# Eight zero blocks issued from ACT's queue instead of SP's, in a fused attention, routed-expert and gated-projection kernel

## The reference

```python
# 1. gated recurrence over 768 steps for 4 x 8 heads of width 40
C = f_stab * C + i_stab * outer(v_t, k_t);  n = f_stab * n + i_stab * k_t
y_t = sigmoid(o_t) * (C @ q_t) / max(|n . q_t|, 1)
# 2. x = y as 3072 tokens x 320; one of 8 experts a token
logits = x @ w_gate;  e_idx = argmax(logits)
out[mask_e] = gate_w * sigmoid(x @ w_output_gate)[e] * (relu(x[mask_e] @ w1[e]) @ w2[e])   # 320 -> 1024 -> 320
# 3. RMS norm, then (silu(xn @ w_gate) * (xn @ w_val)) @ w_out                              # 320 -> 1536 -> 320
```

## Time and profile before

| | us |
|---|---|
| median of 3 runs (863.89 to 868.11) | 866.64 |
| the profiled execution's own time | 862.2 |
| its span, first to last instruction | 860.4 |
| PE busy | 824.9 (96%) |
| DVE busy | 516.9 (60%) |
| ACT busy | 389.3 (45%) |
| POOL busy | 152.1 (18%) |

### The profile page before, as it was taken

One profiled execution on the slowest core, in us unless ns is written; L12 is line 12 of the kernel. 1 busy time (PEld: TensorE's weight loads), 2 busy tenths in 40 slices (PEclk: granted clock), 3 DMA queues, 4 the chain that ended last, 5 costly groups with the idle time before them and its releaser, 6 DMA issues.

```text
span 860.4 us, 18327 instructions
## 1 busy us (share of the span) xinstructions
PE 824.9 (96%) x6220; PEld 742.1 (86%) x6221; DVE 516.9 (60%) x1086; ACT 389.3 (45%) x727; POOL 152.1 (18%) x234
## 2 busy tenths in 40 slices
PE   6999998897999999999999999999999999999994
PEld 3878777696999999999998898888888888888883
DVE  5489876897787787887873353354353354354331
ACT  5455553553777777777752322323223233233221
POOL 3557775630000000000100001001001001001001
PEclk8799998798999999999999999999999999999998
DMA  6667778598989988899921001000100100100000
GB/s 186 147 179 210 209 216 217 179 316 259 298 256 278 284 260 281 250 278 285 321 87 45 1 1 50 19 0 31 37 0 30 37 0 30 37 0 30 1 1 30
DMA packets 74605, 115.72 MB, mean 134 GB/s; under 512 B 10920, under 2 KB 43208, under 8 KB 74552
## 3 DMA queue, kind: packets, MB, share of 16 engines
q1 hardware_dynamic: 71864, 106.37, 42.0%
q0 software_dynamic: 2688, 8.68, 2.8%
HBM read 97.18 MB, written 17.83 MB: 134 GB/s over the span
## 4 chain that ended last, share of the span: by engine, by line
PE 87%; DVE 4%; DMA 3%; issue 2%; SPq 2%; POOL 1%; ACT 0%; POOLq 0%; ACTq 0%; DVEq 0%
PE psum L1556 46%; PE psum L1678 5%; PE psum L1677 5%; PE psum L1676 5%; PE psum L1628 4%; PE psum L1630 4%; PE psum L1629 4%; PE psum L1499 3%; PE psum L1454 3%; PE psum L1475 2%; PE psum L1522 2%; PE psum L1469 1%; PE psum L1513 1%; PE psum L1655 1%; PE psum L1548 1%
## 5 line engine op out<-in xcount | busy, mean ns | idle before, releaser
L1412 DVE TENSOR_TENSOR gated_lo<-gated,gated_hi 128x512 fp32r<-128x512 f32 x72 | 49.9, 693 | 182.2 <-ACT gated_hi L929 182.2
L924 ACT ACTIVATE sigm_sb<-psum 128x512 f32<-128x512 f32 x72 | 43.1, 598 | 249.6 <-PE psum L1556 249.6
L1556 PE MATMUL psum<-nT_hi,w_gv_hi 128*128 128x512 f32 x432 | 122.2, 391 | 1.8 <-DVE nT_lo L1399 1.8
L1556 PE MATMUL psum<-nT_lo,w_gv_hi 128*128 128x512 f32 x432 | 122.0, 391 | 0.0
L1556 PEld LDWEIGHTS psum<-nT_lo,w_gv_hi 128*128 128x128 f32 x432 | 81.2, 188 | 17.8
L754 POOL DMA_INDIRECT out<-out_rows,slot_idx x24 | 23.2, 968 | 389.4 <-ACT out_rows L935 384.0
L1556 PEld LDWEIGHTS psum<-nT_hi,w_gv_hi 128*128 128x128 f32 x432 | 78.6, 188 | 14.4 <-issue 2.1
L1676 PE MATMUL psum<-w_out_hi,gated_hi 128*128 128x320 f32 x288 | 89.2, 310 | 0.0
L1678 PE MATMUL psum<-w_out_hi,gated_lo 128*128 128x320 f32 x288 | 89.1, 309 | 0.0
L1677 PE MATMUL psum<-w_out_lo,gated_hi 128*128 128x320 f32 x288 | 89.0, 309 | 0.0
L1556 PE MATMUL psum<-nT_hi,w_gv_lo 128*128 128x512 f32 x288 | 88.7, 389 | 0.0
(11 more groups left out here) (225 smaller groups left out, 1588.3 us busy)
## 6 DMA issues: line engine op xcount, KB each, us to landing
w_raw<-w SPq DMA_DIRECT2D x38, 640.0 KB, 6.4
w_raw<-w SPq DMA_DIRECT2D x38, 512.0 KB, 4.4
w_raw<-w SPq DMA_DIRECT2D x76, 128.0 KB, 5.0
kv_tok<-tok SPq DMA_DIRECT2D x24, 324.0 KB, 6.1
qk_sb<-qk SPq DMA_DIRECT2D x48, 160.0 KB
x_tile<-x_by_expert SPq DMA_DIRECT2D x12, 386.0 KB, 3.1
y_sorted<-y_tile SPq DMA_DIRECT2D x12, 323.0 KB, 5.2
og_tok<-o_tok SPq DMA_DIRECT2D x24, 160.0 KB, 5.7
```

What stands on the lines that cost most here:

```text
L924: nc.scalar.activation(sigm_sb[f % 2][:], bank[2 * (f % 2)][:], ACT.Sigmoid).then_inc(sig_ready, 1)
L1412: dve.tensor_tensor(gated_lo[f % 4][:], gated[f % 2][:], gated_hi[f % 4][:].bitcast(F32), ALU.subtract).then_inc(hv_lo, 1)
L1556: m = mm(dst, w, x, start=(n == 0), stop=(n == len(terms) - 1))
```

## The change

The eight zero blocks, with the load of the count that each of them needs, leave SP's program and stand in ACT's, between `gate_exp(NC - 1)` and `e_step(0)`. ACT waits for `zero_made` and `cnt_table` ahead of them. What they write, the tile they read and the semaphore `zero_rows` that they increment are the same, and SP's waits for `tables_ready`, `zero_rows` and the scatters stay.

```diff
             x_load(1, TE, row)
             w2_load(1, ex)
-            sp.wait_ge(cnt_table, 1)
-            for e in range(E):
-                n_e = sp.value_load(cnti[0:1, e:e + 1], min_val=0, max_val=NTOK)
-                sp.dma_start(x_by_expert[bass.ds(n_e + e * RS, TE), :].rearrange("(s p) n -> p s n", p=P),
-                             zero[:].unsqueeze(1).to_broadcast([P, TE // P, XW])).then_inc(zero_rows, 16)
             sp.wait_ge(tables_ready, 2)
             sp.wait_ge(zero_rows, 16 * (E + TE // TS))
             rows_scattered(NC - 1)
...
             h_high(0, 0, TE)
             gate_exp(NC - 1)
+            act.wait_ge(zero_made, 2)
+            act.wait_ge(cnt_table, 1)
+            for e in range(E):
+                n_e = act.value_load(cnti[0:1, e:e + 1], min_val=0, max_val=NTOK)
+                act.dma_start(x_by_expert[bass.ds(n_e + e * RS, TE), :].rearrange("(s p) n -> p s n", p=P),
+                             zero[:].unsqueeze(1).to_broadcast([P, TE // P, XW])).then_inc(zero_rows, 16)
```

## The result

The changed kernel takes 872.79 us (median of 10 runs, 868.43 to 877.78) where the kernel before, run beside it, takes 863.75 (860.80 to 868.66). The ratio is 1.0085 with a 95% interval of 1.0062 to 1.0108, so the change costs 7.3 us (5.4 to 9.3). The two medians lie 9.0 us apart, also inside that interval; every cost in this document is worked out from its ratio. The profiled execution took 868.43 us.

A forecast was written before the change was run, and what follows sets the result against it. PE, without idle time from 214 to 430 us, was taken to bound the kernel; 9.7 us of later SP less 1.6 of clock gave 8.1, added to 866.64: forecast 874.7 us, range 870.5 to 881.5.

The forecast's parts named there:

- The loop on ACT as long as SP's, 11.83 us: ACT's eight loads and issues ahead of h_high(0,1) take what SP's took, 11.83 us.
- DVE late by 12.3 us: DVE finishes h_low(0,3) at 197.3 instead of 185.05, so the tables behind it are ready at 206.7.
- SP late by 12.3 - 2.63 = 9.7: SP's wait before tile 2's loads ends 9.7 us later; the threshold, 2.63 us, is how early the tables had been.
- PE's pauses, and the 9.7 us of the sum: New pause of about 10 us in expert_out(0); last pause, before tile 2's work, shrinks to 1.5, ending 9.7 later.
- The clock holds behind the last pause, 1.6 us back: Behind a last pause of only 1.5 us, PE keeps its full clock, which gives back 1.6 us.
- Nothing gives it back: PE's unbroken stretch behind its last pause has no idle time to absorb the delay: 8.1 us later in all.
- the prediction's other branch: PE's clock falls all the same behind the last pause: 876.3 us.
- The rival of a dearer issue on ACT: ACT's issues cost up to POOL's 1008 ns, lengthening the loop by up to 5.1 us: 876.3 to 881.4; chance 0.20.
- The rival of an ACT that isn't held: Issuing is short on ACT or its arithmetic goes on beside it, so the time stays 866.6; chance 0.06.
- with all loads at 272 ns the loop is 1.7 us shorter: Lower bound on ACT's loop: 8 x (479 - 272) = 1.7 us below SP's 11.83.
- The 9.3 us of transfer: Eight zero blocks of 386 KB at 331 GB/s: 9.3 us of transfer, beside 11.83 us of issuing.
- rival 3: In between: a loop of 5 to 8 us on ACT, lateness 2 to 6 us, 869 to 873; chance 0.09.

The follow-up runs named there:

- act_busy: The kernel before, blocks left on SP, with 24 chained copies on ACT where the changed kernel has the blocks; ratio 1.0069 (1.0043 to 1.0095).
- act_busy4: The kernel before, blocks left on SP, with 4 chained copies on ACT where the changed kernel has the blocks; ratio 0.9990 (0.9968 to 1.0012).
- act_busy12: The kernel before, blocks left on SP, with 12 chained copies on ACT where the changed kernel has the blocks; ratio 1.0004 (0.9980 to 1.0028).
- w1_first: First half of tile 2's first weights loaded ahead of the zero-row wait: on the kernel before, ratio 0.9938; on the changed kernel, 1.0081.
- hoist_act: The changed kernel with the eight register loads in a row first, then the eight issues, all on ACT; ratio 1.0095 (1.0058 to 1.0131).
- half_each: The changed kernel with four of the blocks on ACT at the same place and four on SP; ratio 1.0022 (0.9995 to 1.0050).
- act_late: The changed kernel with ACT's eight blocks moved behind w1_high(1,1) of the first step; ratio 1.0004 (0.9972 to 1.0036).
- w1_first_hoist: The kernel before with w1_first's early weights load, and SP's eight register loads in a row ahead of its issues; ratio 1.0010 (0.9988 to 1.0032).
- hoist_sp: The kernel before with SP's eight register loads in a row first, then its eight issues; ratio 1.0021 (0.9996 to 1.0045).

## Why the prediction was right

The forecast was 8.1 us slower, 874.7; measured are 7.3 us (5.4 to 9.3) and 872.79 against a kernel before of 863.75 instead of 866.64. The path through ACT, DVE, the tables and SP was right, step by step. That the clock term came out had luck in it. The steps, each with what it measured:

- **The loop on ACT as long as SP's, 11.83 us.** From 180.24 to 181.14 + 10.79 = 191.93 it is 11.69. The load's median is 552 ns against 479, the issue's 383 against 375. That act_busy delays tables and SP alike with copies shows that the length is enough.
- **DVE late by 12.3 us.** The tables stand 24.90 us behind the counts instead of 12.52: 12.4.
- **SP late by 12.3 - 2.63 = 9.7.** 26.46 instead of 16.74 us: 9.7. The threshold is shown by SP's loads in act_busy4 and act_busy12 (one trace each), the change of the last at SP by the pair of w1_first kernels.
- **PE's pauses, and the 9.7 us of the sum.** About 10 us in expert_out(0): 10.10. `w1_low(1,1)` ended the first weights pause where it was expected (206.91, or 208.64 with the counts as early as in before; expected 208.6). The last pause was to be 1.5 us and was 0.75, because it ended sooner: 37.52 us behind the counts instead of 28.44, which is 9.1 us later and not 9.7. That is the one term of the sum that was mis-sized. The weights took 213.18 - 207.10 = 6.1 us from SP's first issue of them to ACT, where before, and so in the sum, they took 205.84 - 199.13 = 6.7. Why they took 0.6 us less is not shown. It isn't that they start later, for with SP's load as late, act_busy's took 7.1 us; between the traces this time varies from 5.3 (act_busy4) to 7.1.
- **The clock holds behind the last pause, 1.6 us back.** It did: from the pause's end to the finishing line it is 11.3 us, where before had 12.8. So the sum as measured is 9.1 - 1.5 = 7.5. This step was the least safe, and its reason, that the pause is shorter than those that a low clock followed, is not borne out. Among the last pauses alone 1.5 us lies between the two kinds: those of 0.21, 0.75 and 0.96 us (act_busy4, after, act_busy12) were followed by the full clock, those of 1.79, 2.26, 3.19, 4.05 and 4.43 (hoist_act, act_busy, half_each, before, act_late) by the low one. But first weights pauses of 1.70, 1.88 and 2.78 us (hoist_act, act_busy, half_each) kept the full clock, and those of 2.36, 2.66 and 2.74 (after, act_busy12, act_busy4) did not. In these six traces exactly one of the two pauses had the low clock behind it, in before and act_late both had. So the length of a pause alone doesn't tell what the clock does behind it. What decides it no run isolates, and how many of the timed runs of the changed kernel went which way isn't recorded; the 876.3 us of the prediction's other branch lie among them too (868.43 to 877.78).
- **Nothing gives it back.** 637.4 and 637.8 us behind the finishing line.

The rival of a dearer issue on ACT fell with the loop's length. The rival of an ACT that isn't held fell with the 12.76 us of idle time behind the loop. One bound was argued wrongly, though it didn't enter the sum: "with all loads at 272 ns the loop is 1.7 us shorter". hoist_act has such loads and a loop that is 1.3 us longer. It had also been worked out from the median of the loads; the eight loads in the trace add up to 4.46 us, so the same bound would have been 2.3. The 9.3 us of transfer were counted with 386 KB as thousands of bytes; the blocks are 3.16 MB (the queue's row above), 9.6 us at 331 GB/s, which changes no step. And rival 3, a loop of 5 to 8 us, would have cost less than I said: with a hold of 6 us the times show 0.3 us (-1.7 to 2.4), and in its trace a last pause of 0.96 us had the full clock behind it.

## What to carry to other kernels

The issuing of many large DMAs back to back can hold an engine's later instructions for longer than the transfers' own time: here eight of them held ACT or SP for 11.7 to 13.0 us, against 9.6 us of transfer. Put them on a queue whose next instruction nobody waits for, or behind the work that others need, as act_late does at no cost that could be told. Moving a step from an engine that has slack pays only if what the old engine waits for next was waiting for that step; compare the times at which all of its next wait's conditions are met. A load that needs none of a wait's conditions shouldn't stand behind it: lifting the first half of tile 2's first weights over the wait for the zero rows gave 5.4 us.

## What the runs showed of the hardware

- ACT's sequencer takes the same time as SP's for a DMA issue (378 to 453 ns in the changed kernel against 372 to 411 in before) and a little more for a register load (median 552 against 479 ns in the loop). The shortest register load of the counts took 273 ns on ACT (hoist_act) and 263 on SP (w1_first_hoist). A load was as short with the DMA engines at 1.06 of their time, ahead of the first block (before, 181.92 us: 0.27 us).
- ACT's sequencer issued a DMA 0.02 us before the activation ahead of it had begun to compute (act_late), while the activations behind the loop waited for its end.
- Behind several issued blocks, the delay moves to whichever sequencer instruction comes next: loads of up to 0.96 us with 0.38 us issues (before), or 0.28 us loads with issues of up to 1.21 us on ACT (hoist_act) and one of 1.95 on SP (hoist_sp).
- The granted clock stayed at 1.00 behind a pause of PE's of 2.78 us (half_each) and fell to 0.50 behind ones of 1.79 and 2.13 (hoist_act, before): in these traces the length of a pause alone doesn't tell. The low clock cost about 1.5 us: 5.46 against 3.97 us behind the first weights pause (changed kernel, act_busy) and 12.8 against 11.3 behind the last (before, changed kernel), but 14.1 in half_each.
- One execution's trace can differ from the timed median by more than the effect: half_each's finishing line was 6.8 us late in its trace where the runs say 1.9 (-0.4 to 4.3), with the granted clock at 0.91 from 212 to 250 us.
